# Top-k attention with a gated product: groups of 128 tokens and 256 columns, weights split in that order

## What is computed

```python
scores = scale * np.matmul(q, k.transpose(0, 1, 3, 2))      # q, k, v: (4, 8, 576, 64)
kth = np.partition(scores, -32, axis=-1)[..., -32:-31]
attn = softmax(np.where(scores >= kth, scores, -1e9))
x = (attn @ v).transpose(0, 2, 1, 3).reshape(2304, 512)
out = (x @ w_a) * (x @ w_b) @ w_out                          # w_a, w_b: (512, 1536), w_out: (1536, 512)
```

## Time and profile before

| | |
|---|---|
| median of 3 runs | 903.66 us (903.11 to 904.3) |
| profiled execution | 903.46 us |
| its span, first to last instruction | 901.7 us |
| matmul (PE) busy | 830.7 us, 92% |
| weight load (PEld) busy | 744.1 us, 83% |
| DVE busy | 777.1 us, 86% |
| ACT busy | 614.2 us, 68% |
| POOL busy | 472.4 us, 52% |

### The profile page before, as it was taken

How to read it: one execution, slowest core, us unless ns; L and a number is a source line. 1 busy time by engine, 2 the same in 40 slices (tenths; PEclk the granted TensorE clock), 3 DMA queues, 4 the chain that set the end, 5 groups by cost and what they waited for, 6 DMA issues and landing times.

```text
span 901.7 us, 19246 instructions
## 1 busy us (share of the span) xinstructions
PE 830.7 (92%) x6664; PEld 744.1 (83%) x6664; DVE 777.1 (86%) x1668; ACT 614.2 (68%) x1328; POOL 472.4 (52%) x561
## 2 busy tenths in 40 slices
PE   4467678999999999999999999999999999999998
PEld 3355557998899999888999999888999998998897
DVE  3689999997989999989899999988999999997000
ACT  3577777777776777777777776786677777776322
POOL 1667764456545554565454555555454555555232
PEclk9985659999999999999999999999999999999999
DMA  4424651223352232233432322243333222321332
GB/s 111 122 91 131 200 183 52 83 61 87 92 126 66 66 98 74 66 89 94 110 82 76 98 66 65 66 110 86 92 84 102 70 66 71 93 62 54 100 96 75
DMA packets 133008, 81.48 MB, mean 90 GB/s; under 512 B 82224, under 2 KB 109872, under 8 KB 132912
## 3 DMA queue, kind: packets, MB, share of 16 engines
q1 hardware_dynamic: 132368, 80.12, 32.0%
q10 hardware_dynamic: 544, 0.13, 0.1%
HBM read 70.78 MB, written 9.44 MB: 89 GB/s over the span
## 4 chain that ended last, share of the span: by engine, by line
PE 62%; DVE 26%; issue 5%; ACT 4%; DMA 1%; POOL 1%; SPq 1%; ACTq 0%; POOLq 0%
PE ps L473 25%; PE ps L486 13%; DVE work L787 12%; DVE best L770 10%; PE ps L404 6%; PE ps L414 6%; PE ps L437 5%; DVE keep L802 3%; PE ps L363 3%; PE ps L376 2%; ACT k_t L543 1%; DMA k_rows<-in_k 1%; PE ps L429 1%; PE ps L384 1%; ACT scores L580 1%
## 5 line engine op out<-in xcount | busy, mean ns | idle before, releaser
L770 DVE MAX8 best<-work 128x8 f32<-128x576 f32 x432 | 316.7, 803 | 0.0
L707 POOL TENSOR_TENSOR scores<-scores,keep 128x576 f32<-128x576 f32 x144 | 216.4, 1523 | 89.9 <-DVE keep L802 89.9
L473 PE MATMUL ps<-x_hi,w_hi 128*128 128x256 f32 x864 | 250.4, 290 | 1.1 <-ACT x_lo L597 1.1
L473 PE MATMUL ps<-x_lo,w_hi 128*128 128x256 f32 x864 | 243.2, 282 | 0.0
L787 DVE MATCH_REPLACE8 work<-best,work 128x576 f32<-128x576 f32 x288 | 222.7, 798 | 0.0
L473 PE MATMUL ps<-x_hi,w_lo 128*128 128x256 f32 x648 | 182.7, 282 | 0.0
L473 PEld LDWEIGHTS ps<-x_hi,w_hi 128*128 128x128 f32 x864 | 162.8, 188 | 2.9 <-ACT x_lo L597 2.0
L473 PEld LDWEIGHTS ps<-x_lo,w_hi 128*128 128x128 f32 x864 | 162.9, 189 | 0.5
L717 POOL TENSOR_TENSOR h_lo<-ab,h_hi 128x256 fp32r<-128x256 f32 x108 | 79.7, 738 | 128.7 <-ACT h_hi L608 128.6
L572 ACT ACTIVATE scores<-scores,neg_max 128x576 f32<-128x576 f32 x144 | 112.1, 779 | 46.7 <-POOL scores L707 46.6
L713 POOL TENSOR_TENSOR ab<-ab 128x256 f32<-128x256 f32 x108 | 80.1, 742 | 114.1 <-ACT ab L603 111.6
(11 more groups left out here) (52 smaller groups left out, 1331.3 us busy)
## 6 DMA issues: line engine op xcount, KB each, us to landing
wo_lo<-x_scratch SPq DMA_DIRECT2D x108, 256.0 KB, 2.8
wb_lo<-x_scratch SPq DMA_DIRECT2D x108, 128.0 KB, 2.2
stage<-in_w SPq DMA_DIRECT2D x36, 256.0 KB, 2.7
q_rows<-in_q SPq DMA_DIRECT2D x142, 64.0 KB, 2.2
x_scratch<-wo_lo SPq DMA_DIRECT2D x18, 256.0 KB, 2.4
k_rows<-in_k SPq DMA_DIRECT2D x32, 128.0 KB, 2.4
v_rows<-in_v SPq DMA_DIRECT2D x32, 128.0 KB, 2.6
out<-stage SPq DMA_DIRECT2D x15, 256.0 KB, 2.6
```

What stands on the lines that cost most here:

```text
L473: last = mm(ps_ab[:, which, :], w, x[:, g % 2, kb, :], start=(kb == 0 and i == 0), stop=(kb == KB - 1 and i == 2))
L707: V.tensor_tensor(row, row, keep[:, j, :], ALU.add).then_inc(mask_done, 1)
L770: ins = V.max(best[:, u % 2, j, 8 * r:8 * r + 8], src)
```

## The change

The token group shrinks from 256 to 128 (`G = P`, 18 groups) and the block of a and b grows from 128 to 256 columns (`FB` = 2 blocks of 128 at a time, `FC` = 256). A step "a" or "b" is now 2 times 4 times 3 matmuls with 128 moving columns each; a step "o" is still six matmuls with 512 moving columns. There are again 108 triples of steps, 330 steps in all. A group of 128 tokens is ready after `PER` = 4 units, so `MOE0` = 5.

The weights are loaded and split in an order in which the first 512 columns of a, b and the rows of out that belong to them come first (`W_ORDER`, three rounds of 12 chunks); the first four chunks are done in slots -2 and -1, the others four a slot in slots 0 to 7. Each step of the first group waits only for the chunks that it needs. Low parts that don't fit are now subtracted in place in `stage` and stored from there, and the load of the next chunk into that buffer waits for that store. The reloads are 512 KB of `w_out` and 256 KB of `w_b` a block pair.

`k_t` holds five pairs of keys (`KPAIRS`), taken in turn; preps are one slot earlier at three of four places; the orders of tiles of batches 1 and 2 differ; values are loaded one slot earlier. SP's list is interleaved with the steps of the slot.

```diff
-    G = 256
-    GT = G // P
+    G = P
     GROUPS = TOKENS // G
+    FB = 2
+    FG = NF // FB
+    FC = FB * P
+    NCB = DFF // WC
-    RING = 3
+    RING = 2
+    KPAIRS = KB + 1
-    ORDER = [[0, 1, 2, 3, 4], [0, 4, 1, 2, 3], [0, 1, 2, 4, 3], [4, 0, 1, 2, 3]]
+    ORDER = [[0, 1, 2, 3, 4], [4, 0, 1, 2, 3], [0, 1, 2, 3, 4], [4, 0, 1, 2, 3]]
...
-        for p in range(KB):
-            at = last_unit(b - 1, p) - 1
+        for p in range(1, KB):
+            at = last_unit(b - 1, p - 1) - 1
             while at in PREP_AT:
                 at += 1
+            if p == 1:
+                PREP_AT[at - 1] = (b, 0)
             PREP_AT[at] = (b, p)
...
+    W_ORDER = []
+    for cb in range(NCB):
+        W_ORDER += [which * WB0 + kb * NCB + cb for which in range(2) for kb in range(KB)]
+        W_ORDER += [WO0 + cb * (WC // P) + f for f in range(WC // P)]
+    W_CB = WCH // NCB
     STAGES = 3
-    W_AT = {s: list(range(s * W_EACH, (s + 1) * W_EACH)) for s in range(WCH // W_EACH)}
+    W_AT = {}
+    for i in range(WCH):
+        W_AT.setdefault(-2 + i // 2 if i < 4 else (i - 4) // 4, []).append(i)
...
+            def load_w(i):
+                if i < WCH:
+                    wait(sp, w_lo_done, i - STAGES + 1)
+                    wait(sp, st_w[i % STAGES], 16 * stores_of(i))
+                    sp.dma_start(stage[:, i % STAGES, :], w_parts[W_ORDER[i]]).then_inc(ld_w[i % STAGES], 16)
+
+            def store_low(i):
+                n = W_ORDER[i] - LOW
+                sp.wait_ge(w_lo_done, i + 1)
+                sp.dma_start(xs[n * P:(n + 1) * P, :], stage[:, i % STAGES, :]).then_inc(st_w[i % STAGES], 16)
...
             for s in range(FIRST, LAST):
-                for b, p in V_AT.get(s, []):
-                    load_v(b, p)
                 load_q(s + 4)
-                for c in W_AT.get(s, []):
-                    if c >= LOW:
-                        store_wo(c)
-                    load_w(c + STAGES)
-                if s + 1 in PREP_AT and PREPS.index(PREP_AT[s + 1]) > 1:
-                    load_k(PREPS.index(PREP_AT[s + 1]))
+                for part in range(PARTS):
+                    for n in steps_of(s)[part]:
+                        after_step(n)
+                    for i in w_of(s, part, 4) if part < 4 else []:
+                        if W_ORDER[i] >= LOW:
+                            store_low(i)
+                        load_w(i + STAGES)
+                    if part == 0:
+                        for b, p in V_AT.get(s, []):
+                            load_v(b, p)
+                    if part == 2 and s + 1 in PREP_AT and PREPS.index(PREP_AT[s + 1]) > 1:
+                        load_k(PREPS.index(PREP_AT[s + 1]))
...
+                    if F < FG:
+                        pe.wait_ge(w_lo_done, cb * W_CB + (which + 1) * KB)
+                    for i in range(FB):
+                        for kb in range(KB):
+                            at = kb * DFF + (f + i) * P
+                            c, o = which * WB0 + at // WC, at % WC
+                            high = w_hi[:, c, o:o + P]
+                            low = w_lo[:, c, o:o + P] if c < LOW else wb_lo[:, F % RING_B, kb - LKB, i * P:(i + 1) * P]
+                            for m, (w, x) in enumerate(((high, x_hi), (high, x_lo), (low, x_hi))):
+                                last = mm(ps_ab[:, which, i * P:(i + 1) * P], w, x[:, g % 2, kb, :],
+                                          start=(kb == 0 and m == 0), stop=(kb == KB - 1 and m == 2))
```

More of the change, by code:

```diff
@@ L224, in is_tail, with stores_of @@
             return UNITS[u][1] == FULL
+        def stores_of(i):
+            return sum(W_ORDER[n] >= LOW for n in range(i % STAGES, min(i, WCH), STAGES))
         def preps_before(u):
@@ L232, in topk_attention_gated_product @@
             pieces = []
[L233 to L241, removed]
+            tokens = TOKEN_OF[g * G:(g + 1) * G]
+            at = 0
+            while at < G:
+                n = 1
+                while at + n < G and tokens[at + n] == tokens[at] + n:
+                    n += 1
+                pieces.append((at, n, tokens[at]))
+                at += n
             PIECES.append(pieces)
@@ new lines, in store_low, with stored_low @@
+            def store_low(i):
+                n = W_ORDER[i] - LOW
+                sp.wait_ge(w_lo_done, i + 1)
+                sp.dma_start(xs[n * P:(n + 1) * P, :], stage[:, i % STAGES, :]).then_inc(st_w[i % STAGES], 16)
+            def stored_low(cb, of_b):
+                for n in range(STAGES):
+                    last = cb * W_CB + (2 * KB if of_b else W_CB) - 1
+                    while last % STAGES != n:
+                        last -= 1
+                    wait(sp, st_w[n], 16 * (stores_of(last) + (W_ORDER[last] >= LOW)))
@@ L308, in load_wb @@
                              ).then_inc(ld_wb[F % RING_B], 16)
             def store_y(g):
-                wait(sp, y_ready, GT * (g + 1))
-                for t, at, n, row in PIECES[g]:
-                    sp.dma_start(out[row:row + n, :], y[at:at + n, t, :]).then_inc(st_y, 16)
+                sp.wait_ge(y_ready, g + 1)
+                for at, n, row in PIECES[g]:
+                    sp.dma_start(out[row:row + n, :], y[at:at + n, g % 2, :]).then_inc(st_y, 16)
             def after_step(n):
@@ L457, in step @@
                         return
+                    which = 0 if kind == "a" else 1
                     if kind == "a":
-                        if f == 0:
+                        if F % FG == 0:
                             wait(pe, xlo_done, PER * (g + 1))
                         wait(pe, ab_copied, F)
[L462 to L465, removed]
+                    else:
                         wait(pe, ld_wb[F % RING_B], 16 * (F // RING_B + 1))
[L467 to L474, removed]
+                    if F < FG:
+                        pe.wait_ge(w_lo_done, cb * W_CB + (which + 1) * KB)
[8 more added lines that the diff above has]
+                                          start=(kb == 0 and m == 0), stop=(kb == KB - 1 and m == 2))
                     if kind == "b":
@@ L671, in _, with split_lo @@
             V = nc.gpsimd
[L673 to L681, removed]
+            def split_lo(i):
+                pool.wait_ge(w_hi_done, i + 1)
+                c, part = W_ORDER[i], stage[:, i % STAGES, :]
+                to = w_lo[:, c, :] if c < LOW else part.bitcast(fp32r)
+                V.tensor_tensor(to, part, w_hi[:, c, :], ALU.subtract).then_inc(w_lo_done, 1)
             def split_k(n):
```

107 lines of the change are left out of this document (49 added, 58 removed).

## The result

| | before | after |
|---|---|---|
| median | 903.45 us (903.11 to 904.3) | 1153.11 us (1146.83 to 1158.15) |
| ratio | | 1.2758, 95% interval 1.268 to 1.2836 |
| profiled execution, its span | 903.46, 901.7 us | 1149.01, 1147.1 us |
| PE busy | 830.7 us, 92% | 1086.1 us, 95% |
| PEld busy | 744.1 us, 83% | 1014.3 us, 88% |

The medians are of four executions each. The change costs 250 us. One execution further down, the profiled one of split_only (1179.28 us), ran more than 1.5% longer than the fastest of its kernel, and is left out where times are compared.

What follows compares the result with a forecast made beforehand. PE was taken as the bound, DVE just beneath; 91.7 + 761.0 + 256.7 + 16.8 + 8 + 3 + 3 - 4 = 1136.2 us to the last matmul, 1142 us with tail and run offset, range 1112 to 1195.

Steps and rivals of the forecast that it cites:

- main term: Steps a and b: 5184 matmuls of 128 columns for 2592 of 256, +256.7 us.
- PE full, so all of it on the path: Gated product's stage: PE is the bound, so the stream's whole +256.7 us adds to the time.
- 0.109 us a matmul, the load as the reason: Steps a and b: the weight load isn't hidden beside 128 moving columns; 0.109 us each, ends 0.107 and 0.119.
- Rival 1, the load hidden: Steps a and b: each matmul costs 0.06 us, +3 instead of +257, giving 888 us; chance 3%.
- early start: Gated product starts four slots earlier, 44.7 us, at 91.7 us; attention of those slots adds 16.8 us.
- Weights, +3 us: Splits ahead of the first attention and SP's waits for stores before chunk loads: +3 us, between -3 and +15.
- Half clock, +8 us: First steps a and b, slots 5 and 6, meet a low clock: +8 us, between 0 and +20.
- Rival 3, the clock doesn't hold: Gated product's stage: a sixth of PE's work at half clock gives 1310 us, all about 2150; chance 6%.
- Reloads at nothing: Doubled `w_out` reloads, 512 KB, at most about 6 us to land, hidden by more than 13 us; nothing counted.
- Group borders, +3 us: First "a" of each group waits for the last x_lo, 18 groups for 9: +3 us, 0 to +8.
- ACT's waits, -4 us: Longer slots give ACT time, so part of PE's waits for it goes: -4 us, 0 to -10.
- The signs: Profile after: matmuls and loads 0.109 us apart, PEld busiest, DVE 70% of the span, slots 14.1 us.

Runs made afterwards that it cites:

- split_only: The kernel before, each matmul of steps a and b cut into two of 128 columns, each with its own weight load; ratio 1.2871.
- second series: The changed kernel run again unaltered, as control of the later experiments; median 1148.81 us.
- weights_64: The changed kernel with weights of 64 columns in steps a and b, half of the output columns left out; 902.82 us.
- moving_64: The changed kernel with 64 moving columns in steps a and b, half of the tokens left out; 1417.77 us.
- late_load: The changed kernel with each weight chunk's load issued one chunk later; median 1144.12 us.
- late_load_warm: late_load with eight added 512-column matmuls, result unread, in each of slots 3 and 4; 1153.30 us.

## Why the prediction was right, point by point

The forecast was 1142 us with 1112 to 1195; measured were 1153 and, in the second series, 1149. So the main term came out, and the smaller misses partly cancel, as the sum at the end of this section shows. For the end of the last matmul it had 1136.2 us, the trace has 1144.1.

- **PE full, so all of it on the path:** right. From 135 to 1144 us PE is busy 997.62 of 1009 us, and split_only shows the whole loss with nothing else changed.
- **0.109 us a matmul, the load as the reason:** right, and shown by weights_64 and moving_64. The size is a little off: 5.31 / 48 is 0.111, and over two slots (one entry of 5.31, four of 2.63) 15.83 / 144 = 0.110 us. 5184 x 0.001 = +5 us. The rows it came from were a single pair and a stream of another type.
- **Rival 1, the load hidden:** wrong, and its price was wrong too. weights_64 is about that case, with 0.060 us a matmul, and took 903 us instead of 888. The term that failed is the early start, which the sum counted at 44.7 - 16.8 us with only 8 + 3 us off: the start came 4 us later than the sum had it, and PE idled 11 us more behind it where the sum had 1 less. The 8 us for the half clock were right there.
- **Weights, +3 us:** the failing sentence is "half of the chunks are stored, two a slot". On average that is so, but `W_ORDER` puts the six stored ones of each dozen in a row, four of them in one slot. The start came at 97.6 instead of 91.7 + 3. Of the 5.9 us between 91.7 and 97.6, the stores are 3.5 by late_load; the rest stays open.
- **Half clock, +8 us:** the mechanism was right, the size was too small: 12 us. "The denser stream should bring the clock up sooner" is the step that failed. At half clock PE was full and the clock stayed down for 17 us, in late_load_warm for 46. (at 50.26 us, lies ahead of the first entry of the profile's clock at 56.2 us; that it is the lower clock rests on its own 1.30 us, against the 1.14 of five L442 at half clock in moving_64.)
- **Rival 3, the clock doesn't hold:** from 135 us on it held for 1009 us at 128 columns, and at 64 it didn't. But the sign named for this, "a clock row below full after 110 us", did show in a small way: half clock to 114.5 us and from 124.7 to 135.0, and in the slowest execution of split_only for 44.4 us just behind the stream's start. Ahead of these two falls PE had idled a little, 1.3 of 10.2 us and 0.9 of 3.4; in moving_64, at 64 columns, it had hardly idled at all. The rival was near.
- **Reloads at nothing:** wrong once. "More than 13 us later" holds for every block but the last, where only one "o" step lies between:

```profile
1142.42 0.47 PE L516 MATMUL ps<-w_hi,h_hi 128*128 128x512 f32 x1 [2.28 <-DMA wo_lo<-x_scratch]
```

  The load of 512 KB took 4.0 us to land (median), `RING` = 2 left it 1.4 us, and PE stood for 2.3 us.
- **Group borders, +3 us, and ACT's waits, -4 us:** PE itself, in the gated product's stage, waited for x_lo 1.1 us before and 1.9 after, twice each; that is +0.8 rather than +3. (The 3.1 of the earlier trace rows and the 4.3 of after, in six and four places, have the waits of the weight loads in them.) PE's other waits for ACT fell from 14.5 to 10.8 us, -3.7: right. Of the 9.5 us in the earlier trace rows, 8.8 lie in this stage.
- **The signs:** PEld was to be the busiest engine; it is not, by busy time (1014.3 us against PE's 1086.1). The slots of 14.1 us, DVE's 70% and the spacing came out (14.05, 68%, 0.110).
- **Together:** added up from the two traces as for weights_64, between the first and the last matmul of the gated product, in us:

| | before | after | forecast | measured |
|---|---|---|---|---|
| a and b, at full clock | 318.6 | 579.6 | +256.7 | +261.0 |
| attention | 266.3 | 281.5 | +16.8 | +15.2 |
| o | 161.2 | 159.7 | 0 | -1.5 |
| lost to half clock | 0 | 12.0 | +8 | +12.0 |
| PE idle (ACT, x_lo, the reload) | 14.8 | 13.5 | +3 - 4 | -1.3 |
| sum | 760.9 | 1046.3 | +280.5 | +285.4 |

The late start adds 2.9 us to the 5 us of the last row, and these are the 7.9 us between 1136.2 and 1144.1. Too small were the half clock by 4.0, the stream by 4.3, the start by 2.9 and the reload by 2.3; too large were the group borders by 2.2 and the attention by 1.6, and step o took 1.5 less than before.

The Trainium skill, "TensorE: Matmul & The Clock Gate", section "Back-to-back issue gap", has 81 ns for a sustained stream of loads and matmuls with 128 columns. For these fp32r operands the measurement differs and decides: 110 ns. The Trainium skill's rule on the same page, section "LDWEIGHTS (loading the stationary operand)", columns divided by 1.2, gives 107 ns for 128 columns and 53 for 64. The first agrees with the 108 to 111 of the traces; of the second, weights_64 shows only that the load takes no more than the 60 ns between its matmuls.

## What to carry to other kernels

Look at what a load of stationary weights costs beside the matmul that hides it: here 0.11 us against 0.12, so the stream was a hair from load-bound. Halving the moving columns of each matmul doubled the loads, and the loads then set the pace. The price can be read before the change from one pair of instructions, if one compares how long the chain stays on a matmul that follows a narrow one. And work started early is worth only what the clock and the queues that feed it are ready for: 28 us on paper were 10 to 12 here, by the ratios of split_only and the changed kernel.

## What was not expected of the hardware

- A stream of loads with 64 moving columns let the granted clock fall to 0.78 on average over 990 us in which PE was busy for 981; with 128 columns it was 1.00 in the same stretch.
- Once low, the clock stayed low through up to 46 us in which PE was all but full with 128-column matmuls (44.55 of 46.20 us busy in late_load_warm). Once up, it fell again within the stream in after, at 124.7 us, and from 135 us on stayed up for 1009 us.
- Twelve matmuls nobody needed, 2.9 us of work, made the kernel's median 4.6 us faster, though its profiled execution doesn't show how.
